# A fused attention, gated feed-forward and mixing kernel: one pair's normalisation, one product and two loads in other slots

## What is computed

```python
def _attn_ref(q, k, v):
    scores = scale * np.matmul(q, k.transpose(0, 1, 3, 2))
    rel = pos[:, None] - pos[None, :]
    mask_plain = (rel >= 0) & (rel < 32)
    mask_dil = (rel >= 0) & (rel < 128) & (rel % 4 == 0)
    scores = np.where(masks, scores, -1e9)
    attn = np.exp(scores - np.max(scores, axis=-1, keepdims=True))
    attn = attn / (np.sum(attn, axis=-1, keepdims=True) + 1e-09)
    return np.matmul(attn, v)

def _moe_ref(x, mu_k, mu_r, w_k, w_v, w_r):
    xk = mu_k * x + (1.0 - mu_k) * x_prev
    xr = mu_r * x + (1.0 - mu_r) * x_prev
    k = np.maximum(xk @ w_k, 0.0)
    v = k * k @ w_v
    r = 1.0 / (1.0 + np.exp(-(xr @ w_r)))
    return r * v

def _moe2_ref(x, U, V, w_ch1, w_ch2):
    u = x + (x.transpose(0, 2, 1) @ U @ V).transpose(0, 2, 1)
    return u + np.maximum(u @ w_ch1, 0.0) @ w_ch2
```

## Time and profile before

| | us |
|---|---|
| median of 3 runs | 766.21 (765.93 to 768.17) |
| the profiled execution | 765.51 |
| its span, first to last instruction | 763.7 |
| TensorE busy | 732.5 (96%) |
| VectorE busy | 329.6 (43%) |
| ScalarE busy | 302.1 (40%) |
| GpSimd busy | 168.6 (22%) |

### The profile page before, as it was taken

One profiled execution on the slowest core, in us unless ns is written; L12 is line 12 of the kernel. 1 busy time (PEld: TensorE's weight loads), 2 busy tenths in 40 slices (PEclk: granted clock), 3 DMA queues, 4 the chain that ended last, 5 costly groups with the idle time before them and its releaser, 6 DMA issues.

```text
span 763.7 us, 13122 instructions
## 1 busy us (share of the span) xinstructions
PE 732.5 (96%) x4860; PEld 640.6 (84%) x4860; DVE 329.6 (43%) x687; ACT 302.1 (40%) x814; POOL 168.6 (22%) x257
## 2 busy tenths in 40 slices
PE   4799898999999999999999999999999999999998
PEld 3678687888787887788889999998999999899997
DVE  5888767587676726635321312312131231213111
ACT  4786666676677757535441211111121111112110
POOL 6997121212120214304881000000000000000000
PEclk9999899999999999999999999999999999999999
DMA  7875454535444211001442102000110200011001
GB/s 143 203 188 97 104 118 105 105 87 124 105 86 100 70 55 56 1 29 56 138 145 34 42 1 42 31 11 12 29 41 0 41 29 12 12 29 42 0 1 42
DMA packets 165843, 49.00 MB, mean 64 GB/s; under 512 B 142880, under 2 KB 159776, under 8 KB 165792
## 3 DMA queue, kind: packets, MB, share of 16 engines
q1 hardware_dynamic: 129088, 43.99, 23.1%
q10 hardware_dynamic: 36704, 4.34, 3.7%
HBM read 34.98 MB, written 9.37 MB: 58 GB/s over the span
## 4 chain that ended last, share of the span: by engine, by line
PE 82%; DVE 4%; DMA 4%; ACT 4%; SPq 2%; issue 2%; ACTq 1%; POOL 1%; DVEq 0%
PE bank L1371 26%; PE bank L1373 25%; PE bank L1372 25%; DMA probs_t<-probs_dram 2%; PE bank L1429 2%; DMA probs_dram<-probs_blocks 2%; ACT probs L829 1%; ACTq L839 1%; PE bank L1392 1%; PE bank L1520 1%; SPq L627 1%; DVE probs L1165 1%; PE bank L1532 1%; ACT relu_k L914 1%; DVE probs_blocks L1175 1%
## 5 line engine op out<-in xcount | busy, mean ns | idle before, releaser
L1338 DVE SCALAR_TENSOR_TENSOR h_l<-bank,h_h 128x384 fp32r<-128x384 f32 x96 | 53.5, 558 | 289.6 <-ACT h_h L1064 289.6
L1064 ACT ACTIVATE h_h<-bank 128x384 fp32r<-128x384 f32 x96 | 47.2, 491 | 317.8 <-PE bank L1373 317.8
L1373 PE MATMUL bank<-ut_h,w_l 128*128 128x384 f32 x384 | 129.4, 337 | 0.0
L1371 PE MATMUL bank<-ut_h,w_h 128*128 128x384 f32 x384 | 129.3, 337 | 0.0
L1372 PE MATMUL bank<-ut_l,w_h 128*128 128x384 f32 x384 | 128.9, 336 | 0.0
L1373 PE MATMUL bank<-w_h,h_l 128*128 128x512 f32 x288 | 113.7, 395 | 0.0
L1372 PE MATMUL bank<-w_l,h_h 128*128 128x512 f32 x288 | 113.5, 394 | 0.0
L1371 PE MATMUL bank<-w_h,h_h 128*128 128x512 f32 x288 | 112.0, 389 | 0.0
L1371 PE MATMUL bank<-xs_h,wk_h 128*128 128x256 f32 x288 | 83.6, 290 | 1.2 <-DVE xs_l L1188 0.7
L1372 PE MATMUL bank<-xs_l,wk_h 128*128 128x256 f32 x288 | 81.0, 281 | 0.0
L1373 PE MATMUL bank<-xs_h,wk_l 128*128 128x256 f32 x288 | 80.8, 280 | 0.0
(11 more groups left out here) (123 smaller groups left out, 1213.1 us busy)
## 6 DMA issues: line engine op xcount, KB each, us to landing
stage<-in_moe_w_ch_dram SPq DMA_DIRECT2D x16, 512.0 KB, 3.3
out_dram<-result SPq DMA_DIRECT2D x18, 256.0 KB, 2.1
u_tile<-result SPq DMA_DIRECT2D x80, 48.0 KB, 2.0
probs_dram<-probs_blocks SPq DMA_DIRECT2D x12, 240.0 KB, 2.0
probs_t<-probs_dram SPq DMA_DIRECT2D x36, 80.0 KB, 2.2
k_raw<-in_k_dram ACTq DMA_DIRECT2D x64, 40.0 KB, 2.3
q_raw<-in_q_dram SPq DMA_DIRECT2D x64, 40.0 KB, 2.2
q_raw<-in_q_dram SPq DMA_DIRECT2D x64, 32.0 KB, 2.1
```

The source lines that it names most:

```text
L1064: act.activation(h_h[:, m % KRING, :], h_bank[m % 2][:, 0:C2], ACT.Relu).then_inc(hh_done, 1)
L1338: dve.scalar_tensor_tensor(h_l[:, m % KRING, :], h_bank[m % 2][:, 0:C2], 0.0, h_h[:, m % KRING, :].bitcast(F32), op0=ALU.max, op1=ALU.subt ...
L1371: pe.matmul(dst, lhs[0], rhs[0], start=start, stop=False)
L1373: return pe.matmul(dst, lhs[1], rhs[0], start=False, stop=stop)
```

## The change

Four things move; none is added or taken away.

1. `LATER` and `SECOND_ONE` put T of pair 2 in slot 0 of its chunk instead of slot 1. VectorE then normalises and turns pair 2 directly behind the results of the previous chunk and before the square of unit 0; SP's write and reads of that pair come before the values that it loads in slot 0. For this, ScalarE takes both halves of the exponentials before the unit's own relu or sigmoid (`all_exps`), and the copy of a C step in such a slot behind it; there is one such C, of (2,1) in slot 10.
2. `THIRD_ONE` puts A of (3,0) in slot 10 instead of 9.
3. `V_AFTER` of chunks 1 to 6 issues wv product 1 in slot 3, before the visit, instead of in slot 4.
4. SP issues U and V in slot 26 instead of slot 20.

```diff
-LATER = {"A": [-13, -6, -5, -4], "B": [-7, -4, -1, 1], "T": [-5, -2, 1, 4], "D": [-1, 1, 3, 6]}
-THIRD_ONE = dict(LATER, A=[-11, -6, -5, -4])
+LATER = {"A": [-13, -6, -5, -4], "B": [-7, -4, -1, 1], "T": [-5, -2, 0, 4], "D": [-1, 1, 3, 6]}
+THIRD_ONE = dict(LATER, A=[-10, -6, -5, -4])
...
-SECOND_ONE = {"A": [-5, -4, -3, -1], "B": [-4, -3, -1, 1], "C": [-2, 0, None, None], "T": [None, None, 1, 4], "D": [-1, 1, 3, 6]}
+SECOND_ONE = {"A": [-5, -4, -3, -1], "B": [-4, -3, -1, 1], "C": [-2, 0, None, None], "T": [None, None, 0, 4], "D": [-1, 1, 3, 6]}
...
-V_AFTER = [[[], [], [], [], [1], [], [], [2, 3], [4], [5, 6, 7]]] + [[[], [], [], [0], [1], [2], [], [3], [4], [5, 6, 7]]] * (NC1 - 1)
+V_AFTER = [[[], [], [], [], [1], [], [], [2, 3], [4], [5, 6, 7]]] + [[[], [], [], [0, 1], [], [2], [], [3], [4], [5, 6, 7]]] * (NC1 - 3)\
+    + [[[], [], [], [0], [1], [2], [], [3], [4], [5, 6, 7]]] * 2
...
-                if slot == 2 * NUNIT:
+                if slot == 2 * NUNIT + UNIT["k", 4]:
                     load_u()
                     load_piece(PIECE_V)
...
+            def all_exps(slot):
+
+                for k, p in pairs_in("B", slot - 1):
+                    exps(k, p, 0)
+                    exps(k, p, 1)
+                    if MOVED_FROM <= nth(k, p) + RAWS < NPART * PAIRS:
+                        load_keys(*divmod(nth(k, p) + RAWS, PAIRS))
...
                     if soon:
-                        attention_slot(c * NUNIT + n)
+                        all_exps(c * NUNIT + n)
...
-                        if not soon:
+                        if soon:
+                            for step in steps_in(c * NUNIT + n):
+                                attention(*step)
+                        else:
                             attention_slot(c * NUNIT + n)
```

More of the change, by code:

```diff
@@ L839, in load_keys @@
                     act.dma_start(raw_part(k_raw[n % RAWS], k, part), rows_of(k_in, k, p, part)).then_inc(qk_in[n % RAWS], 16)
+            def all_exps(slot):
[4 more added lines that the diff above has]
+                        load_keys(*divmod(nth(k, p) + RAWS, PAIRS))
             def attention_slot(slot):
-                behind = [(k, p) for st, k, p in steps_in(slot - 1) if st == "B"]
+                behind = pairs_in("B", slot - 1)
                 for k, p in behind:
@@ L848, in attention_slot @@
                     exps(k, p, 1)
-                for n in [nth(k, p) + RAWS for k, p in behind]:
-                    if MOVED_FROM <= n < NPART * PAIRS:
-                        load_keys(*divmod(n, PAIRS))
+                    if MOVED_FROM <= nth(k, p) + RAWS < NPART * PAIRS:
+                        load_keys(*divmod(nth(k, p) + RAWS, PAIRS))
             def split_high(n):
```

## The result

| | before | after |
|---|---|---|
| median, us | 766.21 (5 runs, 765.34 to 768.17) | 760.87 (5 runs, 760.19 to 761.59) |
| profiled execution, us | 765.51 | 761.35 |
| its span, us | 763.7 | 759.5 |
| TensorE waits on turned probabilities, 55 to 420 us | 8.9 us in 6 | 6.1 us in 5 |

The changed kernel takes 0.9924 of the time, with a 95% interval of 0.9906 to 0.9943: 5.8 us less by the ratio. The prediction was 759.5 in a range of 752.5 to 763.0.

A forecast was written before the change was run, and what follows sets the result against it. TensorE's instruction stream was taken as the bound. A gain of 13.5 us, less 5.8 for U and V in slot 26 and 1.0 for small waits, gave -6.7 and a median of 759.5 us, range 752.5 to 763.0.

The forecast's parts named there:

- The frame: TensorE's own stream of instructions sets the end; only its idle time and stretches at the lower clock can be won.
- Part 1: Pair 2 normalised and turned ahead of the square on VectorE: the four steps end 1.4 us earlier, at no cost.
- Part 2: A wv product of six matmuls ahead of D(k,2) in slot 3: D(k,2) reached 1.4 us later, at no cost.
- So all six waits end: TensorE's waits at D(k,2), chunks 1 to 6, and two clock falls end: gain 13.5 us including 0.3 for a relu.
- Part 3: U and V in slot 26 on SP: new wait of 3.6 us at D(4,1) plus 2.2 for the clock, cost 5.8.
- Rival (a): U and V's issues in slot 26 fill SP's waiting time, D(4,1) does not wait: 753.7 us, chance 0.25.
- Part 4: Pair 3 gets less time: D(k,3) just fits by 0.7 us, D(k+1,1) may wait; 1.0 us in all, 0 to 3.
- rival (c): Slower: each D(k,3) in six chunks waits 2.6 us and the clock falls, 29 us added: 788 us, chance 0.04.
- the prediction's reading: TensorE's clock fell to half after idle times over 2.5 us and did not fall after 1.47 us.
- eight issues against one trip: SP's 5.2 us for eight issues against 5.06 for a DRAM round trip: the skill's rule does not agree in size.

The follow-up runs named there:

- e4: Kernel before with only pair 2's turn moved ahead of the square and U and V in slot 58, no wv product ahead: 753.91 us, 0.9819.
- e6: Changed kernel with U and V in slot 58 and slot 7's loads of values issued behind slot 8's read back: 753.46 us, 0.9814.
- e7: Changed kernel with U and V issued by GpSimd instead of SP, in about the same slots: 754.92 us, 0.9839.
- e12: Same kernel as e6, measured again beside e9: 754.37 us, ratio 0.9823 to the kernel before.
- e10: Kernel before with only pair 2's turn moved ahead of the square, U and V left in slot 20: 756.55 us, 0.9846.
- e1: Changed kernel with U and V issued in slot 20 again, all else of the change kept: 756.43 us, 0.9851.
- e3: Changed kernel with U and V issued in slot 58 instead of slot 26: 756.14 us, 0.9844.
- e9: Same kernel as e6 but with the wv product no longer put ahead of the visit in slot 3: 758.94 us, 0.9890.
- e5: Changed kernel with U and V in slot 58 and pair 2 turned behind the square as before: 759.34 us, 0.9882.
- e8: Kernel before with only U and V moved, to slot 58: 763.74 us, 0.9951.
- e2: Kernel before with only U and V moved, to slot 26: 765.47 us, 0.9968.

## Why the prediction was right, point by point

**The frame held.** TensorE's stream sets the end, and only its idle time and its low clock were to be won. The kernels at 0.984 or below show it in their profiles. On turned probabilities TensorE waits 2.0 us in e4, 1.3 in e6, 2.9 in e7 and 2.4 in e12. The clock is whole in e4 and e6, and low for 3 to 4 us, once, in e7 and e12.

**Part 1: right in kind, too small in two chunks.** The four steps end 1.5 us earlier against the results in chunk 3 (2.8 instead of 4.26), as I had put at 1.4. But I took chunk 3's value for all. In chunk 1 it is 3.1 by the same count, by VectorE's idle time of 2.15 us ahead of the square. In chunk 2 it is 2.0 (the turn ends 4.97 us after the start of the results before, 2.99 in the changed kernel), and there moving T also moved SP's write and read back ahead of U and V. The prediction counted the queue of VectorE for the moved step, and not its place in SP's program.

**Part 2: the step that failed, without harm to the sum.** "So all six waits end" was argued as 1.4 + 1.4 us against waits up to 2.70. All six ended, but part 1 alone leaves 0.4 of them (e4). Beside part 1, and with the changed kernel's order of loads of values, it brings nothing that these runs can tell: without it and with it the ratios are 0.9846 and 0.9851 (e10, e1), and 0.9819 and 0.9844 (e4, e3). That the sum needed both parts was wrong, and that it came out all the same was luck. It pays where SP's order makes D(k,2) late, as in e9 against e6.

**Part 3: right in place, and in size by two errors that cancelled.** The new wait was forecast at 3.3 to 3.8 us, taken as 3.6, and is 3.96 in one profile and 3.10 in the other. SP took 4.2 us for the eight issues instead of 5.2, and lost more than that, 1.5 us, in the queries behind, for which the prediction had no term. That these two nearly cancel was luck. The clock fell, and cost 2.8 where I had 2.2, the upper end of what I gave. Total 6.8 against 5.8 by the profile; by the ratio of e3, 0.9844, against those of the changed kernel, 0.9924 and 0.9913, it is 6.1 and 5.3 us. Rival (a), that U and V find cover, was wrong: what it would have given, 753.7, is what the kernel reaches when they do leave SP's path (0.9839 and 0.9844 of 766.21 are 753.9 and 754.3).

**Part 4: too small, and for half of it another cause.** I put 1.0 for the small waits, between 0 and 3; they are 2.16. D(k,3) fits within 0.3 us, so rival (c) didn't come. D(5,1) waits 0.57 (1.24 in e3, where D(4,1) doesn't hold TensorE up), and not without part 2 (e4, e10): that is the chain that I worked out. But the wait at D(3,1) stands without part 2 just as well (1.43 in e4, 1.52 in e10). It is not B(k+1,0) coming later. TensorE comes to it 5 us earlier, since the 2.70 and the low clock of chunk 1 are gone (117.04 before, 113.12 - 1.09 after). Its turn ends at 102.80 and no longer at 108.23, but the write is issued at 107.40, only 0.85 us earlier than before, because eight loads of queries and 2.5 us of value loads stand ahead of it. Moving those ended it (e6, e9).

**Sum.** -13.5 + 5.8 + 1.0 became about -13.5 + 6.8 + 2.2 = -4.5 in the profiles. The medians differ by 5.3 and the ratio gives 5.8, of 6.7 forecast: parts 3 and 4 took 2.2 us more than was allowed for, and the short waits of VectorE's making gave 0.7 that was not counted.

**What remains open**: what the longer executions of part 2 alone (e5) waited for ahead of their falls of the clock, and what holds up the landing of the write of (5,2) in e9.

## What to carry to other kernels

When a step moves to another slot, follow every queue in which it stands: moving this turn moved a DRAM write and read past eight loads, which made the separate move of those loads needless, and that move then cost half of what the change had won. A load that nobody needs soon belongs where its queue is idle, or on another engine's queue, and the room must be looked at again after the next move (D(7,2) in e9); whether a wait comes from the queue or from the traffic is told by letting another engine issue the same bytes in the same stretch. Two edits that cover the same wait are measured one at a time, because the first may be enough: part 1 with U and V in slot 58 takes 753.9 us, 1.8% below the kernel before and about 1% below the changed one (by the ratios 0.9819, and 0.9924 and 0.9913), and nothing tried was clearly faster.

## What the runs showed of the hardware

**The clock does not follow the idle time alone.** In these profiles the granted clock went to the lower level, 1.2 of 2.4 GHz, behind waits of 3.96, 3.10, 2.70 and 2.54 us. It also went there behind shorter ones: 2.28 and 2.15 in e8, 2.24 and 1.50 in e2, 1.83 in e12, 1.64 in e7 and 1.62 in e1. The first line is of e8. In e2, behind the second, matmuls of 512 columns take 0.63 us instead of 0.40 from 197 to 200:

```profile
86.79 1.11 PE L1429 MATMUL bank<-probs_t,v_raw 96*64 96x64 f32 x16 [2.28 <-DVE probs L1133]
...
195.63 0.80 PE L1429 MATMUL bank<-probs_t,v_raw 96*64 96x64 f32 x20 [1.50 <-DMA probs_t<-probs_dram]
```

It stayed whole behind 1.94 us in e2, and in e9 behind 1.64 and even 2.82, as the stretch behind D(7,2) shows:

```profile
257.86:260.00 2.14, 2.14 (x26) 1.84 (x27) 1.23 (x5) 0.55 (x1) 0.00 (x0) 1.00 0.40 92
```

In the second profile of the changed kernel D(4,1) itself still ran in 0.68 us behind 3.10 us of idle, and the clock was low only from about 151 on:

```profile
149.50 0.68 PE L1441 MATMUL bank<-probs_t,v_raw 64*64 64x64 f32 x16 [3.10 <-DMA probs_t<-probs_dram]
```

So the prediction's reading, that the clock falls behind idle times of over 2.5 us and not behind 1.47, does not hold in either direction. Behind a wait of 1.5 us or more a fall is possible here and not certain, and the term for it belongs in the range. What decides it these runs don't show.

**An issue's duration is not a constant.** The four issues of V took SP 2.89 us before and 1.89 after; four loads of queries took 1.95, 2.62 or 3.42. What stretches them isn't shown. The Trainium skill, "DMA: Bandwidth & Descriptors", section Issuing engines are not separate DMA queues, calls the sequencer's time to start a DMA usually small relative to the DMA. For one transfer the trace does not contradict this: an issue of U or V took 0.42 to 0.60 us, and the transfer landed about 2.2 us after it. The prediction set eight issues against one trip, which is another comparison. But issues on one queue add up: SP spent 4.2 us on eight, and giving them to GpSimd was worth 0.75 to 0.85% of the kernel.
